# Mixing the first six blocks on VectorE alone, in pairs, and transposing the second tile's x in two halves

## The reference

```python
w = softmax(weight_gen, axis=-1)                 # per token 8 heads x 7 taps
x_pad = six zero rows ahead of each batch's x
x1[s, h, g] = sum_k w[s, h, k] * x_pad[s + k, h, g]      # 8 heads x 24 columns
x2 = (sigmoid(x1 @ w_gate) * (x1 @ w_val)) @ w_out       # 192 -> 1536 -> 192
h  = x2 @ w_in                                           # 192 -> 2048
g  = (a0 + a1 h + a2 h^2 + a3 h^3) / (1 + |b0||h| + |b1|h^2 + 1e-6)
z  = g @ w_out2                                          # 2048 -> 192
```

## Time and profile before

| | us |
|---|---|
| median of three runs | 1369.43 |
| the profiled execution | 1369.59 |
| its span in the trace | 1367.8 |
| TensorE busy | 1332.0 (97%) |
| VectorE busy | 1231.4 (90%) |
| ScalarE busy | 1068.4 (78%) |
| GpSimd busy | 388.0 (28%) |

### The profile page before, as it was taken

One profiled execution on the slowest core, in us unless ns is written; L12 is line 12 of the kernel. 1 busy time (PEld: TensorE's weight loads), 2 busy tenths in 40 slices (PEclk: granted clock), 3 DMA queues, 4 the chain that ended last, 5 costly groups with the idle time before them and its releaser, 6 DMA issues.

```text
span 1367.8 us, 18858 instructions
## 1 busy us (share of the span) xinstructions
PE 1332.0 (97%) x7058; PEld 1208.2 (88%) x7058; DVE 1231.4 (90%) x1520; ACT 1068.4 (78%) x1429; POOL 388.0 (28%) x221
## 2 busy tenths in 40 slices
PE   5999999999999999999999999999999999999977
PEld 4899899889889889899899899899899899899977
DVE  8777989999989999899999999899899998889998
ACT  3487887787788788787787788788787887788986
POOL 4443232232224224132232224224132341200111
PEclk9999999999999999999999999999999999999989
DMA  9200201102121020211102121020211102101000
GB/s 254 68 33 16 66 16 57 42 0 72 27 69 30 12 72 16 71 28 56 43 1 72 28 71 28 20 73 7 69 28 56 39 1 62 28 12 28 12 8 18
DMA packets 46587, 58.49 MB, mean 43 GB/s; under 512 B 5024, under 2 KB 34210, under 8 KB 46496
## 3 DMA queue, kind: packets, MB, share of 16 engines
q1 hardware_dynamic: 46288, 57.06, 14.4%
q10 hardware_dynamic: 144, 0.23, 0.1%
q0 software_dynamic: 64, 0.00, 0.0%
HBM read 39.18 MB, written 16.52 MB: 41 GB/s over the span
## 4 chain that ended last, share of the span: by engine, by line
PE 90%; DVE 3%; ACT 3%; issue 2%; DMA 1%; SPq 0%; DVEq 0%; ACTq 0%
PE ring L449 50%; PE acc L480 39%; ACT work L645 1%; ACT work L653 0%; DVE work L962 0%; PE ring L529 0%; ACT work L642 0%; DVE work L932 0%; ACT work L637 0%; ACT work L643 0%; DVE u L920 0%; DVE work L926 0%; SPq L365 0%; DVE work L939 0%; DVE work L953 0%
## 5 line engine op out<-in xcount | busy, mean ns | idle before, releaser
L480 PE MATMUL acc<-out_w,work 128*128 128x192 f32 x2048 | 365.2, 327 | 3.8 <-DVE work L962 3.8
L480 PEld LDWEIGHTS acc<-out_w,work 128*128 128x128 f32 x2048 | 340.4, 190 | 9.1 <-DVE work L962 4.4
L449 PE MATMUL ring<-yt,in_w 128*128 128x512 f32 (+1 forms) x1360 | 334.8, 387 | 8.7 <-DMA yt<-ys 7.0
L642 ACT ACTIVATE work<-ring,coef 128x512 f32<-128x512 f32 (+1 forms) x256 | 171.6, 670 | 186.0 <-PE ring L449 186.0
L449 PEld LDWEIGHTS ring<-yt,in_w 128*128 128x128 f32 x1360 | 247.4, 191 | 53.6 <-issue 7.5
L480 PE MATMUL acc<-out_w,u 128*128 128x192 f32 x1536 | 282.7, 326 | 5.6 <-DVE u L920 5.6
L799 POOL TENSOR_TENSOR mixed<-mixed,prod 128x768 f32<-128x768 f32 (+1 forms) x90 | 191.9, 2132 | 328.4 <-DVE work L946 322.0
L480 PEld LDWEIGHTS acc<-out_w,u 128*128 128x128 f32 x1536 | 255.7, 190 | 11.7 <-DVE u L920 6.0
L449 PE MATMUL ring<-xt,gate_w 128*128 128x512 f32 (+1 forms) x1020 | 262.3, 387 | 0.8 <-DVE xt L880 0.4
L449 PE MATMUL ring<-xt,val_w 128*128 128x512 f32 (+1 forms) x1020 | 251.6, 377 | 0.0
L449 PEld LDWEIGHTS ring<-xt,val_w 128*128 128x128 f32 x1020 | 185.0, 188 | 35.2
(11 more groups left out here) (74 smaller groups left out, 900.9 us busy)
## 6 DMA issues: line engine op xcount, KB each, us to landing
window<-in_x_dram SPq DMA_DIRECT2D x14, 960.0 KB, 5.1
out_dram<-zsb SPq DMA_DIRECT2D x15, 384.0 KB, 2.5
x_turned<-blocks SPq DMA_DIRECT2D x52, 96.0 KB, 2.0
y_turned<-y_stage SPq DMA_DIRECT2D x52, 96.0 KB, 2.0
xt<-x_turned SPq DMA_DIRECT2D x13, 256.0 KB, 2.7
xt<-x_turned SPq DMA_DIRECT2D x26, 128.0 KB, 2.9
yt<-y_turned SPq DMA_DIRECT2D x13, 256.0 KB, 2.9
yt<-y_turned SPq DMA_DIRECT2D x26, 128.0 KB, 3.0
```

The lines of the kernel that those rows point to most:

```text
L449: last = nc.tensor.matmul(dst, wt[:, c], xs[:, 0:n], start=at == 0, stop=at == 4)
L480: last = nc.tensor.matmul(dst, src[:, n * P:(n + 1) * P], w[:, i, :], start=i == 0 and n % 2 == 0, stop=i == last_i and n % 2 == 1, skip_g ...
L642: nc.scalar.activation(den(n), h, ACT.Abs, scale=coef[:, 6:7])
```

## The change

GpSimd no longer takes part in blocks 0 to 5. VectorE makes all six products and adds up two blocks in one instruction (`early_sum(pair, step)`: 1152, 768 and 384 elements). VectorE's order in quarters k = 1 to 3 is written anew. TensorE's `keep_busy` ahead of the first product goes by product and sum: 3, 3, 2, 2 instead of six times 2. Tile 1's x is copied, transposed and split in two halves of two blocks each; each half's four transposes go into one bank of `acc2`, not the ring, and after the second half five more `keep_busy` matmuls stand. The second X unit is at the end of quarter 3. ScalarE gets the halves' copies between its sigmoids, the second behind piece 12's. SyncE waits for all six products on one semaphore.

```diff
@@ -83,7 +80,8 @@
     NK = 4 * NCH + OFF2 + 4
     LAST = 4 * (NCH - 1) + 1
     def units(k):
-        return TAIL_QUARTER if k >= LAST else QUARTER
+
+        return TAIL_QUARTER if k >= LAST else 'a1212bXab221abbX' if k == 3 else QUARTER
     halves = [("X", 0, 0), ("X", 0, 1)]
     for k in range(NK):
...
@@ -196,23 +194,7 @@
             assert all(w.shape[1] == c0 for w, _ in layers)
         n_pieces = len(pieces)
-
-        taps = [work[:, n:n + K * D].rearrange("p (k d) -> p k d", d=D) for n in (at, at + K * D, 0, K * D)]
-        SPLIT_FIRST = 8
-        assert sum(p[3] for p in pieces[:SPLIT_FIRST]) >= 2 * K * D
-
-        def taps_of(block):
-            return taps[block % 2 + (2 if block in GIVEN else 0)]
-
-        def multiplied(block):
-
-            mine = block in HELPED
-            return (s_taps_g if mine else s_taps_v), sum((t in HELPED) == mine for t in range(block + 1))
-
-        def sums_until(block):
...
@@ -336,14 +320,9 @@
             def load_second_window():
                 sp.dma_start(window[:, HALO + OFFS[1]:ROWS, :], x_rows[:, OFFS[1]:OFFS[2], :]).then_inc(s_window1, 16)
-            def read_until(blocks):
-
-                wait(sp, s_taps_v, sum(t not in HELPED for t in range(blocks)))
-                wait(sp, s_taps_g, sum(t in HELPED for t in range(blocks)))
-
             def load_window(c):
                 if c == EARLY:
-                    read_until(OFFS[EARLY])
...
@@ -453,6 +432,8 @@
                 j, i = divmod(m, F1)
                 wait_bank(pe, "1", m, 0)
                 if i == 0:
+                    if j == 1:
+                        pe.wait_ge(s_half_x, 2)
                     pe.wait_ge(s_x, 2 * j + 2)
                 if j == 0:
                     pe.wait_ge(s_split, pieces_until(w_gate, i * P))
@@ -517,6 +498,19 @@
                 transposes("X", j, lambda n: mixed[:, n, 0:DA],
                            lambda n: x_side[:, n * P:(n + 1) * P], BLOCKS[j]).then_inc(s_xT, 1)
+            def second_x_transposes(half):
+
+                if half == 0:
+                    pe.wait_ge(s_half_twice, 1)
+                else:
+                    pe.wait_ge(s_twice, 2)
+                for n in range(2):
+                    nc.tensor.transpose(acc2[:, half, n * P:(n + 1) * P], mixed[:, 2 * half + n, 0:DA], ident[:, :])
+                for n in range(2, 4):
+                    at = slice((2 * half + n - 2) * P, (2 * half + n - 1) * P)
+                    last = nc.tensor.transpose(acc2[:, half, n * P:(n + 1) * P], x_side[:, at], ident[:, :])
+                last.then_inc(s_xT if half else s_half_xT, 1)
+
             def y_transposes(j):
                 pe.wait_ge(s_ysb, j + 1 - turned(j))
                 transposes("Y", j, lambda n: ysb[:, n * P:(n + 1) * P], lambda n: y_side[:, n * P:(n + 1) * P],
@@ -529,13 +523,15 @@
                     nc.tensor.matmul(bank("1", m, 0)[:, 0:P], ident[:, :], ident[:, :], start=True, stop=True)
             pe.wait_ge(s_ident, 2)
-            pe.wait_ge(s_taps_v, 1)
-            keep_busy(2)
-            for step in range(SUMS * OFFS[1] - 1):
+            for block in range(OFFS[1]):
+                pe.wait_ge(s_taps, block + 1)
+                keep_busy(3)
+            for step in range(SUMS - 1):
                 pe.wait_ge(s_early, step + 1)
                 keep_busy(2)
             x_transposes(0)
             keep_busy(4)
+            xs = 0
             for k in range(NK):
                 m, a, n, b = 3 * k, 3 * k - A_LAG, 4 * (k - OFF2), 4 * (k - OFF2) - B_LAG
                 for unit in units(k):
@@ -556,7 +552,12 @@
                             out2(b)
                         b += 1
                     elif unit == "X":
-                        if k % 4 == 3 and k // 4 + 1 < NCH and k // 4 + 1 not in TURNED:
+                        if k == 3:
+                            second_x_transposes(xs)
+                            xs += 1
+                            if xs == 2:
+                                keep_busy(5, F1)
+                        elif k % 4 == 3 and k // 4 + 1 < NCH and k // 4 + 1 not in TURNED:
                             x_transposes(k // 4 + 1)
                     elif k % 4 == 0 and 1 <= k // 4 <= NCH and k // 4 - 1 not in TURNED:
                         y_transposes(k // 4 - 1)
@@ -579,15 +580,30 @@
                 if j >= NCH or j in TURNED:
                     return
                 if j < EARLY:
-                    act.wait_ge(s_early, sums_until(OFFS[j + 1]))
-                    if j > 0:
-                        act.wait_ge(s_given, SUMS * len(GIVEN))
+                    act.wait_ge(s_early, SUMS * OFFS[j + 1] // 2)
                 else:
                     act.wait_ge(s_mix, MIXES * (j - EARLY + 1))
                 wait(act, s_xT, j - turned(j))
                 n = BLOCKS[j]
                 nc.scalar.copy(x_side[:, 0:n * 2 * DB].rearrange("p (n a d) -> p n a d", a=2, d=DB), mixed[:, 0:n, DA:D].unsqueeze(2).to_broadcast([P, n, 2, DB])
                                ).then_inc(s_twice, 1)
+
+            def second_x_twice(half):
+                act.wait_ge(s_early, SUMS * (OFFS[1] // 2 + half + 1))
+                act.wait_ge(s_xT, 1)
+                at = slice(2 * half, 2 * half + 2)
+                nc.scalar.copy(x_side.rearrange("p (n a d) -> p n a d", a=2, d=DB)[:, at, :, :],
+                               mixed[:, at, DA:D].unsqueeze(2).to_broadcast([P, 2, 2, DB])
+                               ).then_inc(s_twice if half else s_half_twice, 1)
+
+            def second_x_high(half):
+                if half == 0:
+                    act.wait_ge(s_half_xT, 1)
+                else:
+                    act.wait_ge(s_xT, 2)
+                cols = slice(2 * half * P, 2 * (half + 1) * P)
+                for part in range(2):
+                    nc.scalar.copy(xt[1][2 * part][:, cols], acc2[:, half, 2 * part * P:2 * (part + 1) * P]).then_inc(s_xh if half else s_half_xh, 1)
             def x_high(j):
                 if not 0 <= j < NCH:
@@ -700,6 +716,8 @@
             for k in range(LAST):
                 m, n, q = 3 * k, 4 * (k - OFF2), k - OFF2
                 sigmoid(m)
+                if k == 3:
+                    second_x_twice(0)
                 if k == 1:
                     for c in range(10, 12):
                         split_high(c)
@@ -711,11 +729,13 @@
                 hidden(n)
                 if k % 4 == 0:
                     y_copy(k // 4 - 1)
-                if k % 4 == 3:
+                if k % 4 == 3 and k > 3:
                     x_twice(k // 4 + 1)
                 sigmoid(m + 1)
+                if k == 3:
+                    second_x_high(0)
                 hidden(n + 1)
-                if k % 4 == 3:
+                if k % 4 == 3 and k > 3:
                     x_high(k // 4 + 1)
                 if k % 4 == 0:
                     y_high(k // 4 - 1)
@@ -730,6 +750,8 @@
                     exponential((k + 1) // 4 + 2)
                 if k == 3:
                     split_high(12)
+                    second_x_twice(1)
+                    second_x_high(1)
                     split_high(13)
                     split_high(14)
             for k in range(LAST, NK):
...
@@ -834,25 +837,37 @@
                     nc.vector.tensor_tensor(w3, w3, over_k(total[:, 0:n]), ALU.mult).then_inc(s_soft, 1)
             def early_product(block):
-                if block in HELPED:
-                    return
                 c = max(t for t in range(EARLY) if OFFS[t] <= block)
                 if c == 0:
                     dve.wait_ge(s_window0, 48 * B)
                     dve.wait_ge(s_zero, B)
                 else:
                     dve.wait_ge(s_window1, 16)
-                    dve.wait_ge(s_xT, c)
+
+                    dve.wait_ge(s_early, SUMS * (block // 2))
                 dve.wait_ge(s_soft, 6 * (c + 1))
-                tap_products(nc.vector, block).then_inc(s_taps_v, 1)
-
-            def early_sum(block, step):
+                wk = weights(c)[:, (block - OFFS[c]) * HK:(block - OFFS[c] + 1) * HK]
+                nc.vector.tensor_tensor(taps[:, block % 2].rearrange("p k (h g) -> p k h g", g=G),
+                                        window[:, block:block + K, :].rearrange("p k (h g) -> p k h g", g=G),
+                                        wk.rearrange("p (h k) -> p k h", k=K).unsqueeze(3).to_broadcast([P, K, H, G]),
+                                        ALU.mult).then_inc(s_taps, 1)
+
+            def early_sum(pair, step):
+                c = max(t for t in range(EARLY) if OFFS[t] <= 2 * pair)
                 if step == 0:
-                    s, count = multiplied(block)
-                    dve.wait_ge(s, count)
+                    dve.wait_ge(s_taps, 2 * pair + 2)
+                    nc.vector.tensor_tensor(taps[:, :, 0:3, :], taps[:, :, 0:3, :], taps[:, :, 3:6, :],
+                                            ALU.add).then_inc(s_early, 1)
+                    return
```

(71 more changed lines are left out.)

35 lines of the change are left out of this document (11 added, 24 removed).

## The result

| | before | after |
|---|---|---|
| median of seven runs, us | 1369.43 (1369.07 to 1371.85) | 1364.81 (1364.45 to 1365.52) |
| profiled span | 1367.8 | 1362.7 |
| `in1(0)` starts | 20.49 | 17.93 |
| `in1(12)` starts | 50.57 | 45.69 |
| `in2(0)` starts | 64.17 | 59.30 |

The ratio on record, with its 95% interval, is 0.9959 (0.995 to 0.9969). It isn't the quotient of the two medians, which is 0.9966. By the medians the kernel is 4.6 us faster, and the forecast was 1364.8. The spans of the two profiled executions differ by more, 5.1 us, so a span says no more about a median than to some 0.5 us.

The account below looks back on a forecast made before the run. VectorE's list was taken to bound the kernel before `in1(12)`. By TensorE's books, 2.4 us earlier start plus 3.4 fewer waits less 1.1 of new idle matmuls gave 4.7, so 1364.8 us, range 1363.4 to 1367.4.

Parts of the forecast that it names:

- The bound and the method: Before `in1(12)`: VectorE's list is the bound; three instruction lists laid out by hand, good to about 0.1 us.
- 1.34, 0.94 and 0.56 for a pair sum: VectorE's paired sum steps of 1152, 768 and 384 elements, priced by a line through trace durations; 2.84 us a pair.
- 1.95 for a pair of splits: VectorE's two 768-column low parts of weights: 1.95 us without GpSimd beside them, where the trace had 3.51 and 4.19.
- The wait before the second half: TensorE ahead of the transposes of the second half of tile 1's x: a wait of 1.5 us.
- The upper bound of a pair (3.32): VectorE's pair sums costing twice the single steps, 3.32 us; as a rival: gain 3.2, 1366.2 us, chance 0.09.
- TensorE's waits are given as 3.2 in the sum: TensorE's waits before `in1(12)` fall from 6.6 to 3.2 us, listed as 0.9, 0.4, 1.5 and 0.3.
- GpSimd as the cause, the rule of locking: Before `in1(12)`: GpSimd's SBUF reads lock out two-input VectorE instructions; without them stretched ones return to their price alone.
- Costed at nothing: Around tile 1's x: five idle matmuls (1.1 us uncovered), early transposes, copies and load waits hide behind other work, adding nothing.
- the clock as a rival for the first products alone: `in1(0)` and `in1(1)` run at TensorE's low clock level: gain 2.6, 1366.9 us, chance 0.12.
- the halving of x: Tile 1's x: only half its work stands behind the last sum, four 256-column instructions in 1.5 us.
- The 4.7 reach the end: From `in1(12)` to the kernel's end: all starts come 4.7 us earlier, so the whole gain arrives.
- nothing with a fixed date behind 50 us: Behind 50 us: loads done by 38, later work released by engine events, so nothing holds back the 4.7 us.

Follow-up runs that it names:

- a_single: The changed kernel with each pair-sum step made as two instructions, one per block; median 1366.86 us, ratio 0.9976 to the kernel before.
- a_reads: The changed kernel with idle multiplies that read SBUF given to GpSimd at its old places; median 1375.38 us, ratio 1.0039 to the kernel before.
- a_writes: The changed kernel with idle memsets, which only write SBUF, given to GpSimd at its old places; median 1364.94 us, ratio 0.9968 to the kernel before.
- b_keep: The kernel before with GpSimd out of blocks 0 to 5 and 18 idle matmuls ahead of tile 1's x transposes; median 1368.54 us, ratio 0.9988.
- a_together: The changed kernel with both halves of tile 1's x done together at the second half's place; median 1364.78 us, ratio 0.9962 to the kernel before.
- a_nokeep0: The changed kernel without any matmul on the identity ahead of the first product; median 1368.93 us, ratio 0.9993 to the kernel before.

## Why the prediction was right, by its steps

**The bound and the method.** Right. The three lists, with VectorE's as the bound, laid out with durations from the trace, gave 18.0, 30.3 and 45.9 for `in1(0)`, `in1(6)` and `in1(12)`; measured 17.93, 30.15 and 45.69.

**The prices.** 1.34, 0.94 and 0.56 for a pair sum: measured 1.36, 0.96 and 0.56. 1.95 for a pair of splits: 1.95. The wait before the second half: 1.5, measured 1.48. The upper bound of a pair (3.32) was wrong as the price of singles: it added up lone instructions, and a_single shows 3.11 (2.48 and 0.63). TensorE's waits are given as 3.2 in the sum and add up to 3.1 in the brackets behind it; and 1369.43 less 4.7 is 1364.7, not 1364.8. Neither slip matters at the 0.5 us that the measurement resolves.

**GpSimd as the cause, the rule of locking.** Right, shown by a_reads and a_writes, and by the softmax multiply, which took 0.62 when it began first and 2.86 when it didn't. The Trainium skill (SBUF — State Buffer, "Who interferes with whom") says that a VectorE instruction with two SBUF inputs contends with a GpSimd one that reads SBUF, not with one that only writes it; both halves of that agree with 4.03 and 1.95 us.

**"Costed at nothing": wrong in two places, without an effect on the sum.** The five matmuls on the identity were costed as 1.1 us of hidden work. They are no cost but what keeps the clock up: without them `in2(0)` is 1.3 us late, and the time was 1368.0, outside the range, though not all of that is theirs. The sum had no reason to count on them: this part is luck. I had the clock as a rival for the first products alone and never asked which later wait the change lengthens. In that rival the short times were put at 16.2; they came by 15.9. And the halving of x, described as leaving only half of the work behind the last sum, is worth nothing.

**"The 4.7 reach the end": right for this pair, wrong as a rule.** Of the 4.88 us at `in1(12)`, 4.62 stand near 1226 us; TensorE waits 0.3 us more than before between 60 and 80 us:

```profile
60.00:80.00 20.00, 19.97 (x110) 1.00 0.04 11
60.00:80.00 20.00, 19.68 (x113) 1.00 0.10 29
```

(before, after; TensorE alone). Behind 1226 us it took 137.5 before and 137.1 after, so the gain came through. But the other kernels with the same late lists took 136.7 to 139.6 there. What was argued as "nothing with a fixed date behind 50 us" leaves out the clock in the last waits and short waits near 1255. That the two came out alike wasn't foreseen. That is luck, worth up to 2.5 us. Had they fallen as in a_single, the time would have been near 1367, within the range, but for a reason that isn't in it.

**Shares of the gain at `in1(12)`.** 50.57 to 48.61 is GpSimd's leaving with the clock kept up (b_keep); 0.55 is the pair sums (a_single); 0.0 the halving (a_together). The remaining 2.4 us (48.61 to 45.69, less 0.55) are what is left: the place of x's transposes behind `in1(11)` and `out1(10)` and out of the ring, VectorE's new order, and the new order of products, sums and matmuls on the identity ahead of the first product (`in1(0)` at 18.45 in b_keep, 17.93 in the changed kernel). These weren't tried apart, so for this half of the gain the cause is argued from the layout and not shown.

## What to carry to other kernels

Where the list of one engine sets a stretch, lay it out with durations of the trace, and look whether a helper beside it stretches its instructions: here GpSimd's help cost VectorE more than it did (7.9 us of stretching for 5.9 us of work). Look at every wait of TensorE that an edit makes or lengthens, and at the granted clock behind it, before counting matmuls on the identity as waste. And compare kernels at a place behind the edit as well as at the end, since the end can add or hide up to 3 us of its own (136.7 to 139.6 us here).

## What the runs showed of the hardware

- A low clock of TensorE came behind waits that were short: 1.47 and 0.97 us with 1.5 of work between (granted 0.66 in the next 5 us), while in the kernel before one of 2.45 us, with work around it, left it at 1.00. What decides between the two isn't settled here.
- Up to about 15.5 us the granted clock reads 1.00 while the records take twice their later time (20 in 4.77 us, then 8 in 1.06). The column doesn't show the low level at the start; the records do. How long after the first matmul they become short varies: by 15.88 after 11.09 in the changed kernel, 6.7 us in a_nokeep0, and 8.5 us in a_reads, which began at 12.27, had a wait of 1.03 on the way, and at 19.23 still took 1.75 for 8.
- GpSimd's `memset`, 20 in 15.9 us, cost VectorE nothing (1.55 and 1.95 us beside it), its multiplies doubled the splits (4.03), and ten of GpSimd's own multiplies took 21.9 us.
- Two products in a row overlap by some 0.08 us (3.02 for two, 1.55 each), and so do two of `gated` (0.76, 0.42 each). The dependent steps of a sum don't (12.45 + 1.36, the next at 13.84), and neither do two splits of 768 columns, though they don't depend on each other (1.95, 0.96 each). What makes the difference isn't shown.
